# A tuned fp32r kernel: the first piece's columns carried across by engines instead of DMA, a softmax moved up, two narrow banks lifted before they are added

## What is computed

```python
w = exp(weight_gen - max(weight_gen)); w = w / (sum(w) + 1e-9)
conv[b, s, h, g] = sum over k of w[b, s, h, k] * x_pad[b, s + k, h, g]
h = conv.reshape(16384, 192) @ w_in
out = (h * sigmoid(1.702 * h)) @ w_out
```

## Time and profile before

| | us |
|---|---|
| median of 3 runs | 1140.81 |
| the profiled execution, its own time | 1141.14 |
| span of the profiled execution | 1139.4 |
| PE busy in it | 1107.2 (97%) |
| DVE busy | 801.9 (70%) |
| ACT busy | 601.3 (53%) |
| weight loads (PEld) busy | 914.1 (80%) |

### The profile page before, as it was taken

The page is one execution under the profiler, slowest core; times in us unless marked ns, Lnnn a source line. Parts: engine busy times, 40 slices in busy tenths (PEclk is TensorE's granted clock), DMA queues, the critical chain, the costliest instruction groups (busy, mean ns, idle before and its releaser), DMA issues.

```text
span 1139.4 us, 21543 instructions
## 1 busy us (share of the span) xinstructions
PE 1107.2 (97%) x9728; PEld 914.1 (80%) x9728; DVE 801.9 (70%) x674; ACT 601.3 (53%) x629; POOL 0.2 (0%) x4
## 2 busy tenths in 40 slices
PE   1999999999999999999999999999999999999998
PEld 1887888888888888888888888888888888888886
DVE  8896967849577694867849587595876949678322
ACT  3546446464555546455564555645556464564543
POOL 0000000000000000000000000000000000000000
PEclk9999999999999999999999999999999999999999
DMA  7801010100101001010100101001010010100000
GB/s 226 256 15 53 1 39 29 39 29 1 55 12 40 29 6 62 1 39 29 39 29 1 39 29 39 29 2 64 4 39 29 30 38 1 40 29 1 29 1 29
DMA packets 9563, 42.80 MB, mean 38 GB/s; under 512 B 1088, under 2 KB 2752, under 8 KB 7168
## 3 DMA queue, kind: packets, MB, share of 16 engines
q1 hardware_dynamic: 9056, 41.03, 11.1%
q10 hardware_dynamic: 416, 0.39, 0.1%
HBM read 24.12 MB, written 12.58 MB: 32 GB/s over the span
## 4 chain that ended last, share of the span: by engine, by line
PE 92%; DVE 6%; DMA 1%; ACT 1%; issue 0%; ACTq 0%; DVEq 0%; SPq 0%
PE hid L426 43%; PE acc_main L444 29%; PE acc_rest L444 19%; DVE prod L296 2%; DVE conv L303 1%; DVE gate_lo L386 1%; DMA xt<-xt 1%; DVE prod L328 0%; ACT xt L214 0%; ACT gate_hi L247 0%; DVE outs_rest L373 0%; DMA taps<-in_tap_runs 0%; ACT gate L244 0%; DVE conv L296 0%; DVE xt L334 0%
## 5 line engine op out<-in xcount | busy, mean ns | idle before, releaser
L244 ACT ACTIVATE gate<-hid 128x1024 f32<-128x1024 f32 x256 | 263.0, 1027 | 499.3 <-PE hid L426 499.1
L386 DVE TENSOR_TENSOR gate_lo<-gate,gate_hi 128x1024 fp32r<-128x1024 f32 x256 | 312.2, 1220 | 281.9 <-ACT gate_hi L247 281.9
L426 PE MATMUL hid<-xt,w_hi 64*128 64x512 f32 x3072 | 433.7, 388 | 25.9 <-DMA xt<-xt 23.9
L426 PEld LDWEIGHTS hid<-xt,w_hi 64*128 64x128 f32 x3072 | 289.0, 185 | 87.4 <-DMA xt<-xt 23.6
L444 PE MATMUL acc_main<-gate_hi,w 64*128 64x512 f32 x2048 | 315.7, 386 | 0.0
L247 ACT ACTIVATE gate_hi<-hid 128x1024 fp32r<-128x1024 f32 x256 | 261.1, 1020 | 0.0
L444 PEld LDWEIGHTS acc_main<-gate_hi,w 64*128 64x128 f32 x2048 | 192.1, 184 | 40.1
L426 PE MATMUL hid<-xt,w_lo 64*128 64x512 f32 x1536 | 216.8, 387 | 0.0
L444 PE MATMUL acc_rest<-gate_hi,w 64*128 64x512 f32 x1024 | 199.7, 386 | 0.8 <-DVE outs_rest L377 0.8
L444 PE MATMUL acc_main<-gate_lo,w 64*128 64x512 f32 x1024 | 199.5, 386 | 0.0
L444 PE MATMUL acc_rest<-gate_lo,w 64*128 64x512 f32 x1024 | 199.5, 386 | 0.0
(11 more groups left out here) (25 smaller groups left out, 166.9 us busy)
## 6 DMA issues: line engine op xcount, KB each, us to landing
xwin<-in_x_runs SPq DMA_DIRECT2D x15, 1056.0 KB, 5.0
out<-outs_main SPq DMA_DIRECT2D x15, 512.0 KB, 2.6
out<-outs_rest SPq DMA_DIRECT2D x15, 256.0 KB, 2.9
taps<-in_tap_runs SPq DMA_DIRECT2D x1, 3136.0 KB, 20.0
taps<-in_w_rows SPq DMA_DIRECT2D x2, 1536.0 KB, 10.1
w_hi<-w_hi SPq DMA_DIRECT2D x2, 768.0 KB, 8.9
w_lo<-w_lo SPq DMA_DIRECT2D x2, 768.0 KB, 12.4
xt<-xt SPq DMA_DIRECT2D x6, 192.0 KB, 4.0
```

What stands on the lines that cost most here:

```text
L244: nc.scalar.activation(gate[:, v % 2, :, :], hid[:, v % 2, :, :], ACT.Gelu_apprx_sigmoid).then_inc(gate_ready, 1)
L386: nc.vector.tensor_tensor(gate_lo[:, v % SLOTS, :, :], gate[:, v % 2, :, :], gate_hi[:, v % SLOTS, :, :], ALU.subtract).then_inc(gate_lo_r ...
L426: last = nc.tensor.matmul(hid[:, v % 2, h, :], w[rows, k, q, f], xt[rows, j % 2, part, k, :], start=(i == 0), stop=(i == len(terms) - 1))
```

## The change

Five parts. (1) Piece 0 is no longer spread by DMA: ACT copies the upper rows' turned columns into the lower rows of xt, with rounding (hi_crossed), DVE copies the lower rows' rounded columns into the upper rows (hi_crossed), and two subtractions on DVE write the remainders into the other half's rows (lo_crossed). PE waits for both. The spreads of piece 1 stay. (2) SP's and ACT's queues lose piece 0's spreads, so that SP reaches the doubling of the weights without them. (3) `EARLY_AT`: the 4 softmax steps of piece 2 stand in unit 5 of piece 0, between the turn and the split of piece 1, and no longer in unit 6 behind the split; 2 convolution steps follow in unit 6 and 1 in unit 7. (4) `CONV_AT[1]` is (2, 1, 2, 2, 2, 1, 0, 0), and piece 2 is turned in unit 5 of piece 1 instead of unit 6. (5) `evict` of a narrow piece first copies acc_main's second bank and adds acc_rest's, as for wide pieces, which frees the banks, and then adds the halves from SBUF to SBUF (four adds); ACT lifts bank 0 instead of bank 1; the stores wait for main_summed and rest_summed. Beside this DVE gets waits on its own earlier signals ahead of the second multiplication of a piece.

```diff
@@ -23,5 +23,5 @@
-CONV_AT = ((5, 3, 3, 3, 3, 0, 0, 0), (1, 2, 2, 1, 2, 2, 0, 0), (0, 0, 0, 5, 2, 1, 2, 1, 2, 2, 1, 1, 0, 0, 0, 0))
-EARLY_AT = (0, 0, 0, 0, 0, 0, 5, 2)
-TURN_AT, ROUND_AT, SPLIT_AT = (5, 6, 11), (5, 6, 12), (5, 6, 13)
+CONV_AT = ((5, 3, 3, 3, 3, 0, 0, 0), (2, 1, 2, 2, 2, 1, 0, 0), (0, 0, 0, 5, 2, 1, 2, 1, 2, 2, 1, 1, 0, 0, 0, 0))
+EARLY_AT = (0, 0, 0, 0, 0, 4, 2, 1)
+TURN_AT, ROUND_AT, SPLIT_AT = (5, 5, 11), (5, 6, 12), (5, 6, 13)
@@ -136,7 +138,9 @@
-        def spread(eng, j, part, to):
-            there, here = (LOWER, UPPER) if to == 0 else (UPPER, LOWER)
-            return eng.dma_start(xt[there, j % 2, part, :, HALF_N:N].bitcast(F32),
-                                 xt[here, j % 2, part, :, 0:HALF_N].bitcast(F32))
+        def other(there, part):
+            return xt[there, 0, part, :, HALF_N:N]
+        def spread(eng, part, there, here):
+            return eng.dma_start(xt[there, 1, part, :, HALF_N:N].bitcast(F32),
+                                 xt[here, 1, part, :, 0:HALF_N].bitcast(F32))
@@ -155,7 +159,2 @@
-            sp.wait_ge(xt_hi_ready, 1)
-            spread(sp, 0, 0, 0).then_inc(xt_hi_spread, 16)
-            sp.wait_ge(xt_lo_ready, 1)
-            spread(sp, 0, 1, 0).then_inc(xt_lo_spread, 16)
             sp.wait_ge(w1_hi_ready, 1)
@@ -172,5 +171,5 @@
                 if is_narrow(j):
-                    sp.wait_ge(main_out_dve, j + 1)
+                    sp.wait_ge(main_summed, 2 * (j + 1))
                     sp.dma_start(out[0:P, cols], outs_main[:, 0, :]).then_inc(main_stored, 16)
-                    sp.wait_ge(rest_out, 2 * (j + 1))
+                    sp.wait_ge(rest_summed, 2 * (j + 1))
                     sp.dma_start(out[P:D, cols], outs_rest[:, 0, :]).then_inc(rest_stored, 16)
@@ -190,7 +189,7 @@
             sp.wait_ge(xt_hi_ready, 2)
-            for to in range(2):
-                spread(sp, 1, 0, to).then_inc(xt_hi_spread, 16)
+            spread(sp, 0, LOWER, UPPER).then_inc(xt_hi_spread, 16)
+            spread(sp, 0, UPPER, LOWER).then_inc(xt_hi_spread, 16)
             sp.wait_ge(xt_lo_ready, 2)
-            for to in range(2):
-                spread(sp, 1, 1, to).then_inc(xt_lo_spread, 16)
+            spread(sp, 1, LOWER, UPPER).then_inc(xt_lo_spread, 16)
+            spread(sp, 1, UPPER, LOWER).then_inc(xt_lo_spread, 16)
             store(0)
@@ -221,6 +220,3 @@
             round_piece(0)
-            act.wait_ge(xt_hi_ready, 1)
-            spread(act, 0, 0, 1).then_inc(xt_hi_spread, 16)
-            act.wait_ge(xt_lo_ready, 1)
-            spread(act, 0, 1, 1).then_inc(xt_lo_spread, 16)
+            nc.scalar.activation(other(LOWER, 0), turned(0)[UPPER], ACT.Copy).then_inc(hi_crossed, 1)
             exponentials(1)
@@ -231,4 +227,3 @@
                 wait(act, main_stored, 16 * j)
-                h = 1 if is_narrow(j) else 0
-                nc.scalar.activation(outs_main[:, h, :], acc_main[:, h, :], ACT.Copy).then_inc(main_out_act, 1)
+                nc.scalar.activation(outs_main[:, 0, :], acc_main[:, 0, :], ACT.Copy).then_inc(main_out_act, 1)
                 act.wait_ge(rest_added, UNIT0[j + 1])
@@ -293,2 +288,6 @@
                     dve.wait_ge(conv_op, base + (SOFTMAX_STEPS if k <= 2 else q))
+                    if k == 1:
+                        wait(dve, xt_lo_ready, j)
+                        if j == 1:
+                            dve.wait_ge(lo_crossed, 2)
                     to = acc if k == 0 else prod[:, k % 2, 0:u * CB]
@@ -344,3 +343,8 @@
             w1_remainder(slice(0, 2 * P))
+            dve.wait_ge(xt_hi_ready, 1)
+            nc.vector.tensor_copy(other(UPPER, 0), own(0, 0)[LOWER].bitcast(F32)).then_inc(hi_crossed, 1)
             split_piece(0)
+            for there, here in ((LOWER, UPPER), (UPPER, LOWER)):
+                nc.vector.tensor_tensor(other(there, 1), turned(0)[here], own(0, 0)[here], ALU.subtract
+                                        ).then_inc(lo_crossed, 1)
             maxima_and_shift(1)
@@ -357,15 +361,3 @@
                 wait(dve, main_stored, 16 * j)
-                if not is_narrow(j):
-                    nc.vector.tensor_copy(outs_main[:, 1, :], acc_main[:, 1, :]).then_inc(main_out_dve, 1)
-                    for h in range(2):
-                        dve.wait_ge(rest_crossed, 2 * j + h + 1)
-                        nc.vector.tensor_tensor(outs_rest[:, h, :], acc_rest[0:HALF, h, :], outs_rest[:, h, :], ALU.add
-                                                ).then_inc(rest_out, 1)
-                    return
-                first, second = slice(0, HALF_N), slice(HALF_N, N)
-                dve.wait_ge(main_out_act, j + 1)
-                nc.vector.tensor_tensor(outs_main[:, 0, first], acc_main[:, 0, first], outs_main[:, 1, second], ALU.add)
-                nc.vector.tensor_tensor(outs_main[:, 0, second], acc_main[:, 0, second], outs_main[:, 1, first], ALU.add
-                                        ).then_inc(main_out_dve, 1)
+                nc.vector.tensor_copy(outs_main[:, 1, :], acc_main[:, 1, :]).then_inc(main_out_dve, 1)
                 for h in range(2):
@@ -373,7 +365,15 @@
                     nc.vector.tensor_tensor(outs_rest[:, h, :], acc_rest[0:HALF, h, :], outs_rest[:, h, :], ALU.add
-                                            ).then_inc(rest_summed, 1)
-                dve.wait_ge(rest_summed, 2 * (j + 1))
-                for to, of in ((first, second), (second, first)):
-                    nc.vector.tensor_tensor(outs_rest[:, 0, to], outs_rest[:, 0, to], outs_rest[:, 1, of], ALU.add
                                             ).then_inc(rest_out, 1)
+                if is_narrow(j):
+                    halves = ((slice(0, HALF_N), slice(HALF_N, N)), (slice(HALF_N, N), slice(0, HALF_N)))
+                    dve.wait_ge(main_out_act, j + 1)
+                    dve.wait_ge(main_out_dve, j + 1)
+                    dve.wait_ge(rest_out, 2 * (j + 1))
+                    for to, of in halves:
+                        nc.vector.tensor_tensor(outs_main[:, 0, to], outs_main[:, 0, to], outs_main[:, 1, of], ALU.add
+                                                ).then_inc(main_summed, 1)
+                    for to, of in halves:
+                        nc.vector.tensor_tensor(outs_rest[:, 0, to], outs_rest[:, 0, to], outs_rest[:, 1, of], ALU.add
+                                                ).then_inc(rest_summed, 1)
@@ -392,6 +392,6 @@
                     convolve(j + 1, CONV_AT[kind(j)][v])
-                    if j == 0:
-                        convolve(2, EARLY_AT[v])
                     if v == TURN_AT[kind(j)]:
                         turn_piece(j + 1)
+                    if j == 0:
+                        convolve(2, EARLY_AT[v])
                     if v == SPLIT_AT[kind(j)]:
@@ -412,11 +412,13 @@
                     if v == 0 and i == 0:
-                        if is_narrow(j):
-                            pe.wait_ge(xt_hi_spread, 32 * (j + 1))
-                        else:
-                            pe.wait_ge(xt_hi_ready, j + 1)
+                        pe.wait_ge(xt_hi_ready, j + 1)
+                        if j == 0:
+                            pe.wait_ge(hi_crossed, 2)
+                        elif j == 1:
+                            pe.wait_ge(xt_hi_spread, 32)
                     if v == 0 and i == 2 * SLICES:
-                        if is_narrow(j):
-                            pe.wait_ge(xt_lo_spread, 32 * (j + 1))
-                        else:
-                            pe.wait_ge(xt_lo_ready, j + 1)
+                        pe.wait_ge(xt_lo_ready, j + 1)
+                        if j == 0:
+                            pe.wait_ge(lo_crossed, 2)
+                        elif j == 1:
+                            pe.wait_ge(xt_lo_spread, 32)
                     if n in (0, 2) and i == SLICES:
```

More of the change, by code:

```diff
@@ L98, in ffn_of_dynamic_conv @@
         w1_doubled = sem("w1_doubled")
+        hi_crossed, lo_crossed = sem("hi_crossed"), sem("lo_crossed")
         xt_hi_spread, xt_lo_spread = sem("xt_hi_spread"), sem("xt_lo_spread")
@@ L109, in ffn_of_dynamic_conv @@
         main_out_act, main_out_dve = sem("main_out_act"), sem("main_out_dve")
-        rest_crossed, rest_summed, rest_out = sem("rest_crossed"), sem("rest_summed"), sem("rest_out")
+        rest_crossed, rest_out = sem("rest_crossed"), sem("rest_out")
+        main_summed, rest_summed = sem("main_summed"), sem("rest_summed")
         main_stored, rest_stored = sem("main_stored"), sem("rest_stored")
@@ L392, in _ @@
                     convolve(j + 1, CONV_AT[kind(j)][v])
+                    if v == TURN_AT[kind(j)]:
+                        turn_piece(j + 1)
                     if j == 0:
                         convolve(2, EARLY_AT[v])
-                    if v == TURN_AT[kind(j)]:
-                        turn_piece(j + 1)
                     if v == SPLIT_AT[kind(j)]:
```

## The result

The changed kernel takes 1138.76 us (median of 12 runs, 1138.61 to 1138.89), the kernel before in the same comparison 1141.28 (12 runs, 1140.29 to 1144.3). The ratio is 0.9975, 95% interval 0.9967 to 0.9983: 0.25% faster. 1139.0 was predicted, in a range of 1137.7 to 1140.9. The absolute time is 0.2 us off, but the gain is 2.5 us by the medians and not 1.8. The interval (0.17% to 0.33% faster) holds the 0.2% line within it. The profiled execution took 1138.69 (span 1136.9), 2.45 us less than the profiled execution of before.

What follows compares the result with a forecast made beforehand. PE was taken as busy without a gap from 200 to 1100 us, so only stalls before about 115 us could be saved. 1.1 (piece 2) + 0.7 (banks) = 1.8 us off 1140.81 gave 1139.0, range 1137.7 to 1140.9.

Steps and rivals of the forecast that it cites:

- Start of PE at 20.5, little kept: Start of piece 0: first matmul 3.1 us earlier, but waits for gate_hi and gate_lo leave only 0.4 us.
- The delay of DVE, 2.5: DVE's start: cast of 0.50 and three instructions of 0.96 make the maxima and what follows 2.5 us later.
- The lower bound of 2.15: DVE's start: smallest delay of the maxima, 2.15 us, if all four instructions overlap.
- the crossings overlap: Rival, DVE's start and evict: delay 2.15 instead of 2.5 and evict doesn't wait; 1138.3 us, chance 0.30.
- Half rate: Rival, DVE's start: crossed subtractions take 1.9 us each, delaying the whole chain; 1142.3 us, chance 0.07.
- The spread of piece 1 at 58.0: Piece 1: spread comes 1.15 us later, PE's first weight load at 58.0 instead of 56.85, stall grows to 2 us.
- No lo stall in unit 8: Piece 1's start: PE does not wait for the lo spreads, though their split comes later; bound 1.2 us.
- Piece 2 1.1 earlier: Turn of piece 2 on DVE ends 1.1 us earlier, at 91.55; PE's first load at 93.2 instead of 94.27.
- The banks, 0.7: acc_rest is freed earlier: the stall at 106.68 goes, worth 0.7 us; that at 68.92 goes but counts nothing.
- The forecast of 1.8 us: Whole kernel: total gain of 1.8 us, from 1.1 at piece 2 and 0.7 at the banks.
- Late lo spreads: Rival, unit 8: lo spreads land at 60.3, PE waits 1.2 us, only 0.7 is left; 1140.1 us, chance 0.17.
- the cast at 0.96: DVE's start: upper bound for the cast, 0.96 us instead of 0.50, making the delay 3.0 us.

Runs made afterwards that it cites:

- the longer stall: Kernel before, with PE's first load of piece 1 waiting for the lo spreads as well as the hi spreads; 1141.45 us beside 1141.16.
- changed, again: The changed kernel run once more with nothing altered, on another chip; 1138.78 us beside 1141.79 for the kernel before, profiled execution 1140.4.
- hi crossed by the engines: Changed kernel with only piece 0's hi columns crossed by ACT and DVE, its lo columns spread by DMA; 1136.82 us, 1136.8 when repeated.

## Why the prediction was right, and where not

- *Start of PE at 20.5, little kept*: right (20.44). The wait for gate_hi ended at 29.23, forecast 29.1; gate_lo 0 ended at 32.30, forecast 32.15. Of the 0.4 us that I left in hand 0.1 was there (32.45 against 32.55), since PE began the second product only at 32.45, not at 32.15. PE's first matmuls were slow again, 2.81 us for the first 12 against 2.72 before, where 12 later ones take 1.36; the granted clock reads 1.00 there in both traces, so they show no cause. My 27.5 for two units was 20.5 plus before's 9.0 us for 54 matmuls less 18 at 0.1133; the last of them ended at 27.17.
- *The delay of DVE, 2.5*: undersized. It was 2.8: the cast took 0.69 and not 0.50 (the row of the like kind gave too steep a fall), and the instructions left 0.02 to 0.04 between them. The lower bound of 2.15, which needed overlaps, is refuted, and with it the rival *the crossings overlap*. That the gain by the medians is that rival's 2.5 us is luck: its mechanism was not there. Its reason was misread, too: not each pair of DVE rows at the start overlapped before, since an addition that ended at 9.28 was followed at 9.32. *Half rate* is refuted as well (two crossed subtractions in 1.94).
- *The spread of piece 1 at 58.0*: wrong, 56.67. I moved the whole chain of the earlier trace rows by 1.15, and with it the landing time. The spreads took 2.8 to 3.0 us from issue to landing instead of 3.0 to 4.6, and the window's load 4.5 to 4.7 instead of 5.0 to 6.4:

```profile
DMA to landing us min/median/max: 2.8/2.9/3.0
```

```profile
DMA to landing us min/median/max: 4.5/4.6/4.7
```

  Part of this is luck. The bulk load of the taps, issued at 31.2 here and 28.5 before, landed in 15.3 us instead of 20.0. I had costed the move of SP's queue at nothing, and this load does follow it: 15.3 to 16.1 us in the four traces of kernels without GpSimd that issue the doubling of w_in's hi part early, 19.2 to 20.2 in the eight that issue it late; the pair that differs in this alone has 16.1 and 19.2. The window's load does not follow it: 4.6 us with the late doubling in the trace of the longer stall, 5.4 with the early one in two traces, and 7.4 and 5.3 in two executions of one and the same kernel. What made it land quickly here stays open.
- *No lo stall in unit 8*: 0.69, between my 0 and the bound 1.2. It was one of my own signs of being wrong. Since the hi part came 1.3 earlier and DVE still decided at piece 2 (0.99 of idle there), it cost nothing at the end.
- *Piece 2 1.1 earlier*: 1.5 after the 0.16 of the start is taken off. The evict was sized about right: 3.36 us of DVE against 2.92 with the idle time before, 0.44 more where I had 0.54. The missing 0.4 arose between the turn of piece 1 and the first multiplication of piece 2, which I had at 56.3 behind the window's landing and which was at 55.94; gate_lo 8 behind it was as much earlier (62.08, forecast 62.5).
- *The banks, 0.7*: right. Unit 20's lo loads stand at 110.79 and 113.18: 2.39 earlier, against 1.67 at the start of piece 2.
- *The forecast of 1.8 us*: it was too small, and that the time came out within 0.2 us is in part luck: the median that I started from, 1140.81 of three runs, was low by 0.5 (twelve runs gave 1141.28), and the gain was too small by 0.7. By the two profiled executions, neither with a low clock, the gain is 2.45 us, of which the loads show 1.67 at piece 2 and 0.72 at the bank: the term that was undersized is piece 2, 1.1. By the medians it is 2.5, with late runs of before in it: the kernel before has runs up to 4 us above its lowest, the changed one none in the first twelve, and I took the sum over to the medians as if both spread alike. By the lowest runs the gain is 1.7 (1140.29 to 1138.61). This agrees with 1.8, but before's fastest run is 0.85 us faster than its profiled execution, and no trace of such a run shows where.
- *The range*: its upper end does not follow from its terms. Late lo spreads (1140.1) with the cast at 0.96, 0.46 more, make 1140.6 and not 1140.9.
- *What it did not see*: that the crossing is the losing part. Its own steps said that the start keeps 0.4 us and that the chain behind it moves by 1.15; drawn together per part, they would have said that order and banks alone are better.

## What to carry to other kernels

Before an engine takes over a transfer, look at what is queued behind the new instructions on that engine: here 2.6 us of work let the first matmul go 3.1 us earlier, and yet the first second product came 0.4 us later than without the crossing (32.45 against 32.05), the load of piece 1 0.9 and that of piece 2 1.3. Split such a change by its parts and price each alone, and in pairs: the banks gave nothing alone and 0.3 to 0.6 us behind the order. The version with the lowest median took the two copies and left the two subtractions to the DMA. And compare whole distributions of runs: here the medians gained 0.8 us more than the lowest runs.

## What the runs showed of the hardware

- Beside GpSimd's subtractions with two inputs in SBUF, two of DVE's additions that take 1.95 us took 8.28 and 6.12 us in the two traces. The longest addition took 5.27 instead of 0.95 and ended 0.8 us after the subtraction beside which it had begun.
- After stalls of 2.54, 3.31 and 3.68 us PE's granted clock read 0.50 for 3.4 us; after 2.35 us (before), 2.54 us (changed) and 3.01 us (changed, again) it stayed at 1.00. A stall of that length may cost it or not.
- The first 12 matmuls of the span took 2.72 us before and 2.81 in the changed kernel, where 12 later ones take 1.36 (the first six weight loads 0.93 and 0.96, later ones 0.56), although the record of the granted clock shows 1.00 there.
- Behind a DVE instruction on other rows, the split, the crossed subtractions and the reduction each began 0.02 to 0.04 us after its end (changed kernel; hi crossed by the engines). The same reduction right behind the split, on the same rows, began 0.09 us before its end (before; hi crossed by the engines). That the change of rows is the cause is not shown.
- GpSimd's subtraction of 2048 columns took 4.49 and 5.29 us in the two traces, beside DVE's additions, against 2.29 us on DVE.
- A bulk load of 3136 KB took 15.3 to 16.1 us to land where two copies of 768 KB had been issued 16 to 20 us before it, and 19.2 to 20.2 where they were issued 6 to 8 us before it.
